# Attention, rational MLP and gated MLP on one core: first q and k loads of one row tile, q's norms summed on columns, and a new order inside the slots of token block 1

## What is computed

```python
qn = q / (norm(q, axis=1) + 1e-06)          # norms over the 6016 rows, one per column
kn = k / (norm(k, axis=1) + 1e-06)
s = kn.transpose(0, 2, 1) @ qn / tau        # 256 x 256
a = softmax(s)                              # the sum has 1e-9 added
x = v @ a                                   # 6016 x 256
h = x @ w_in                                # 6016 x 2048
P = a0 + a1 h + a2 h^2 + a3 h^3
Q = 1 + |b0| |h| + |b1| h^2
y = (P / (Q + 1e-6)) @ w_out                # 6016 x 256
out = (sigmoid(y @ w_gate) * (y @ w_val)) @ w_out2
```

## Time and profile before

| what | value |
|---|---|
| time before, median of 3 runs | 1206.06 us (1205.66 to 1206.26) |
| the profiled execution | 1205.5 us, of which 1203.7 us is its span |
| around the span | 1.8 us |
| PE busy | 1191.9 us, 99% of the span |
| DVE, ACT, POOL busy | 88%, 73%, 21% |
| granted TensorE clock, mean | 1.000 |

### The profile page before, as it was taken

The page is one execution under the profiler, slowest core; times in us unless marked ns, Lnnn a source line. Parts: engine busy times, 40 slices in busy tenths (PEclk is TensorE's granted clock), DMA queues, the critical chain, the costliest instruction groups (busy, mean ns, idle before and its releaser), DMA issues.

```text
span 1203.7 us, 19532 instructions
## 1 busy us (share of the span) xinstructions
PE 1191.9 (99%) x6772; PEld 1165.5 (97%) x6772; DVE 1064.7 (88%) x1369; ACT 881.3 (73%) x1267; POOL 253.8 (21%) x152
## 2 busy tenths in 40 slices
PE   9998999999999999999999999999999999999998
PEld 8876999999999999999999999999999999999998
DVE  7799999899999989999998999899898989989843
ACT  6898778677777868777786877778687777768632
POOL 0432212112121212212121211212121221212110
PEclk9999999999999999999999999999999999999999
DMA  9820000000000000000000000000000000000000
GB/s 368 300 66 13 1 14 14 13 13 0 13 13 13 13 13 13 0 13 13 13 13 13 13 0 13 13 13 13 13 13 0 13 13 13 13 0 13 0 14 14
DMA packets 15866, 33.81 MB, mean 28 GB/s; under 512 B 1382, under 2 KB 6246, under 8 KB 15846
## 3 DMA queue, kind: packets, MB, share of 16 engines
q1 hardware_dynamic: 14982, 32.51, 7.5%
q10 hardware_dynamic: 864, 1.05, 0.3%
HBM read 27.39 MB, written 6.16 MB: 28 GB/s over the span
## 4 chain that ended last, share of the span: by engine, by line
PE 90%; DVE 5%; DMA 2%; SPq 1%; issue 1%; ACT 1%; DVEq 0%; ACTq 0%
PE ps L905 17%; PE ps L903 17%; PE ps L904 17%; PE ps L1017 7%; PE ps L1018 7%; PE ps L1019 7%; PE ps L1056 5%; PE ps L1058 5%; PE ps L1057 5%; DMA kq<-in_q 2%; PE ps L917 1%; SPq L340 1%; SPq L342 1%; PE ps L940 1%; DVE work L875 0%
## 5 line engine op out<-in xcount | busy, mean ns | idle before, releaser
L453 POOL TENSOR_TENSOR g_parts<-work,g_parts 128x752 fp32r<-128x752 f32 x120 | 218.7, 1822 | 814.4 <-ACT g_parts L634 814.4
L624 ACT ACTIVATE work<-ps,neg_a 128x752 f32<-128x752 f32 x120 | 117.6, 980 | 143.5 <-PE ps L905 82.1
L903 PE MATMUL ps<-v_hi,m_hi 128*128 128x376 f32 x512 | 174.1, 340 | 1.2 <-DVE work L862 1.0
L905 PE MATMUL ps<-v_hi,m_lo 128*128 128x376 f32 x512 | 171.5, 335 | 0.0
L904 PE MATMUL ps<-v_lo,m_hi 128*128 128x376 f32 x512 | 170.4, 333 | 0.0
L1017 PE MATMUL ps<-g_parts,w_hi 128*128 128x376 f32 x480 | 160.7, 335 | 0.0
L1018 PE MATMUL ps<-g_parts,w_hi 128*128 128x376 f32 x480 | 160.0, 333 | 0.0
L1019 PE MATMUL ps<-g_parts,w_lo 128*128 128x376 f32 x480 | 159.4, 332 | 0.0
L748 DVE TENSOR_TENSOR work<-work,ps 128x376 f32<-128x376 f32 x192 | 103.7, 540 | 52.6 <-PE ps L905 39.8
L856 DVE TENSOR_TENSOR work<-work,ps 128x752 f32<-128x752 f32 x120 | 112.0, 934 | 37.7 <-ACT work L627 36.0
L660 ACT ACTIVATE work<-work,consts 128x752 f32<-128x752 int32 x118 | 108.4, 918 | 38.7 <-DVE work L875 38.7
(11 more groups left out here) (131 smaller groups left out, 2862.8 us busy)
## 6 DMA issues: line engine op xcount, KB each, us to landing
work<-in_v SPq DMA_DIRECT2D x16, 376.0 KB, 2.9
out<-work SPq DMA_DIRECT2D x15, 376.0 KB, 2.3
kq<-in_k SPq DMA_DIRECT2D x9, 512.0 KB, 13.2
kq<-in_q SPq DMA_DIRECT2D x9, 512.0 KB, 15.5
before<-in_moe_w_out SPq DMA_DIRECT2D x5, 512.0 KB, 12.6
before<-in_moe_w_in SPq DMA_DIRECT2D x8, 256.0 KB, 7.1
before<-in_moe_w_gate SPq DMA_DIRECT2D x2, 512.0 KB, 9.5
before<-in_moe_w_val SPq DMA_DIRECT2D x2, 512.0 KB, 6.7
```

Source lines behind the costliest of these rows:

```text
L453: nc.gpsimd.tensor_tensor(g_lo[n], g[n], as_f32(g_hi[n]), ALU.subtract).then_inc(g_lo_ready, 1)
L624: nc.scalar.activation(poly[n], h, ACT.Identity, scale=neg_a[:, 3:4], bias=neg_a[:, 2:3])
L903: nc.tensor.matmul(dst, l_hi, r_hi, start=(begins and n == 0), stop=False)
L905: last = nc.tensor.matmul(dst, l_lo, r_hi, start=False, stop=(ends and n == len(parts) - 1))
```

## The change

1. `KQ_SIZES` becomes six chunks of one tile, one of two, one of three, nine of four: 17 chunks. ACT still issues the first six q chunks, which are now six tiles and not eight. The coefficients are issued behind the chunk of two tiles, and are spread before the same tile as before.
2. `norms()` moves four late scores back (`NORMS_AT` = 37) and puts q's norms on columns as well: four narrow products instead of two narrow ones and a wide one. ACT takes one root of 128 x 4. DVE adds the guard to q's two columns, takes their reciprocals, and multiplies the identity matrix by each column (two 128 x 128 products). PE spreads the diagonal over all partitions with a product by ones (`spread_q`, before late score 40), and DVE copies the row out of PSUM.
3. In slots 2 to 6 of block 1, `times_value(*second)` moves from the end of DVE's slot to right behind L862, ahead of `split_gated` and `quad`; and `gate(*second)` moves on ACT ahead of L641.
4. In slots 2 to 7 of block 1 ACT computes |h| before the polynomial's start, and so waits for g only after |h|.

```diff
-    KQ_SIZES = [1] * 4 + [2] * 2 + [4] * ((NT - 8) // 4)
-    KQ_SIZES[6:6] = [NT - sum(KQ_SIZES)]
+    KQ_SIZES = [1] * 6 + [2] + [4] * ((NT - 8) // 4)
+    KQ_SIZES[7:7] = [NT - sum(KQ_SIZES)]
...
-    COEF_SPREAD_BEFORE = 9
+    COEF_SPREAD_BEFORE = 10
...
-    NORMS_AT, TURN_AT = NT - 14, NT - 2
+    NORMS_AT, SPREAD_AT, TURN_AT = NT - 10, NT - 7, NT - 2
...
+        def second_ahead(i, j, second):
+            return is_block(i, 1) and second is not None and j < PAIRS - 1
...
             act.wait_ge(norms_summed, 1)
-            nc.scalar.activation(q_inv, ps_qnorm, ACT.Sqrt).then_inc(norms_squared, 1)
-            nc.scalar.activation(k_norm, ps_knorm, ACT.Sqrt).then_inc(norms_squared, 1)
+            nc.scalar.activation(norms_kq, ps_norms, ACT.Sqrt).then_inc(norms_squared, 1)
             act.wait_ge(norms_squared, 1)
-            nc.scalar.activation(q_inv, q_inv, ACT.Identity, bias=norm_guard).then_inc(norms_rooted, 1)
-            act.wait_ge(norms_squared, 2)
...
                     if now is not None:
+                        h = hidden_of(i, j)
                         act.wait_ge(h_done, now + 1)
...
+                        if is_block(i, 1) and j >= 2:
+                            wait_count(act, quad_ready, now)
+                            nc.scalar.activation(ab, h, ACT.Abs)
+                            act.wait_ge(g_ready, now - 1)
+                            nc.scalar.activation(poly[n], h, ACT.Identity, scale=neg_a[:, 3:4],
+                                                 bias=neg_a[:, 2:3]).then_inc(h_read, 1)
...
+                    if second_ahead(i, j, second):
+                        gate(*second)
...
+            dve.wait_ge(norms_squared, 1)
+            link(nc.vector.tensor_scalar(q_inv, q_inv, 1e-6, None, ALU.add))
+            link(nc.vector.reciprocal(q_inv, q_inv))
+            dve.wait_ge(ident_ready, 1)
+            for c in range(CC):
+                nc.vector.tensor_scalar(q_diag[:, c, :], ident[:], q_inv[:, c:c + 1], None,
+                                        ALU.mult).then_inc(q_diag_ready, 1)
             dve.wait_ge(norms_rooted, 1)
-            link(nc.vector.reciprocal(q_inv, q_inv))
-            dve.wait_ge(norms_rooted, 2)
             link(nc.vector.reciprocal(k_inv, k_norm))
...
                 if c == 0:
+                    dve.wait_ge(q_row_ready, 1)
+                    link(nc.vector.tensor_copy(q_row, ps_qrow))
                     dve.wait_ge(first_scores, 1)
...
+                    if second_ahead(i, j, second):
+                        times_value(*second)
                     if j > 0 and left is not None:
                         split_gated(*left)
...
+            def spread_q():
+                pe.wait_ge(q_diag_ready, CC)
+                nc.tensor.matmul(ps_qrow, ones[:], q_diag.rearrange("p a b -> p (a b)"), start=True,
+                                 stop=True).then_inc(q_row_ready, 1)
```

More of the change, by code:

```diff
@@ L163, in attention_rational_gated_kernel @@
         assert 4 * KQ_W <= 6 * PW
-        q_inv = region(6 * PW, (C,))
+        q_row = region(6 * PW, (C,))
+        q_diag = region(6 * PW + 5 * C, (CC, P))
         att = region(6 * PW + C, (CC, C))
@@ L176, in attention_rational_gated_kernel @@
         neg_min, row_sum, row_inv = small[:, 6:8], small[:, 8:10], small[:, 10:12]
+        norms_kq, q_inv = small[:, 12:16], small[:, 14:16]
         consts = sb("consts", [P, 7])
@@ L189, in attention_rational_gated_kernel @@
         ps_kq = ps[:, 0:2, 0:C]
-        ps_knorm, ps_qnorm = ps[:, 2, 0:CC], ps[:, 3, 0:C]
+        ps_norms, ps_qrow = ps[:, 2, 0:2 * CC], ps[:, 5, 0:C]
         ps_coef = ps[:, 4, 0:7]
@@ L204, in attention_rational_gated_kernel @@
         norms_summed, norms_rooted, small_step = sem("norms_summed"), sem("norms_rooted"), sem("small_step")
+        q_diag_ready, q_row_ready = sem("q_diag_ready"), sem("q_row_ready")
         scores_ready, exps_ready, row_inv_ready = sem("scores_ready"), sem("exps_ready"), sem("row_inv_ready")
@@ L506, in _ @@
             act.wait_ge(norms_summed, 1)
-            nc.scalar.activation(q_inv, ps_qnorm, ACT.Sqrt).then_inc(norms_squared, 1)
-            nc.scalar.activation(k_norm, ps_knorm, ACT.Sqrt).then_inc(norms_squared, 1)
+            nc.scalar.activation(norms_kq, ps_norms, ACT.Sqrt).then_inc(norms_squared, 1)
             act.wait_ge(norms_squared, 1)
-            nc.scalar.activation(q_inv, q_inv, ACT.Identity, bias=norm_guard).then_inc(norms_rooted, 1)
-            act.wait_ge(norms_squared, 2)
             act.wait_ge(coefs_ready, 1)
-            nc.scalar.activation(k_norm, k_norm, ACT.Identity, scale=neg_tau,
+            nc.scalar.activation(k_norm, norms_kq[:, 0:CC], ACT.Identity, scale=neg_tau,
                                  bias=neg_tau_guard).then_inc(norms_rooted, 1)
@@ L620, in step @@
                     if now is not None:
+                        h = hidden_of(i, j)
                         act.wait_ge(h_done, now + 1)
[L622 to L627, removed]
+                        if is_block(i, 1) and j >= 2:
[4 more added lines that the diff above has]
+                                                 bias=neg_a[:, 2:3]).then_inc(h_read, 1)
+                        else:
+                            act.wait_ge(g_ready, now - 2 if is_block(i, 1) and j < 2 else now + (-1))
+                            nc.scalar.activation(poly[n], h, ACT.Identity, scale=neg_a[:, 3:4],
+                                                 bias=neg_a[:, 2:3])
+                            wait_count(act, quad_ready, now)
+                            nc.scalar.activation(ab, h, ACT.Abs).then_inc(h_read, 1)
                     if old is not None and not unsplit(old):
@@ L652, in step @@
                     gate_first = is_block(i, 1) and second is not None
-                    if gate_first:
+                    if gate_first and not second_ahead(i, j, second):
                         gate(*second)
@@ L732, in _ @@
                 link(nc.vector.scalar_tensor_tensor(out=att[:, c, :], in0=ps_kq[:, c, :], scalar=k_inv[:, c:c + 1],
-                                                    in1=q_inv, op0=ALU.mult, op1=ALU.mult))
+                                                    in1=q_row, op0=ALU.mult, op1=ALU.mult))
                 nc.vector.tensor_reduce(neg_min[:, c:c + 1], att[:, c, :], AX_X, ALU.min).then_inc(scores_ready, 1)
@@ L887, in step @@
                         split_gated(*early)
-                    if second is not None:
+                    if second is not None and not second_ahead(i, j, second):
                         times_value(*second)
@@ L923, in norms @@
                 pe.wait_ge(summed, 2 * (len(KQ_CHUNKS) + 3))
[L924 to L928, removed]
+                for n in range(2 * CC):
+                    acc, c = (k_acc, q_acc)[n // CC], n % CC
+                    last = nc.tensor.matmul(ps_norms[:, n:n + 1], acc[:, 0, c * P:(c + 1) * P], ones[:, 0:1],
+                                            start=True, stop=True)
+                last.then_inc(norms_summed, 1)
+            def spread_q():
+                pe.wait_ge(q_diag_ready, CC)
+                nc.tensor.matmul(ps_qrow, ones[:], q_diag.rearrange("p a b -> p (a b)"), start=True,
+                                 stop=True).then_inc(q_row_ready, 1)
             def spare_products(count, dst=ps_spare):
@@ L964, in _ @@
                     norms()
+                if late == SPREAD_AT:
+                    spread_q()
                 if late == TURN_AT:
```

## The result

| | median, us | lowest to highest | ratio to before, 95% interval |
|---|---|---|---|
| before (7 runs) | 1205.75 | 1205.42 to 1206.26 | |
| after (7 runs) | 1210.22 | 1209.78 to 1210.90 | 1.0039 (1.0029 to 1.0048) |
| predicted | 1204.6 | 1203.6 to 1208.0 | |

The change makes the kernel 0.4% slower, and the time lies outside the predicted range. The profiled execution took 1210.9 us, 1209.1 of them its span, 5.4 us more than the span of before. It is the longest of the seven, and its mean granted clock, 0.997, is the lowest (0.998 or 0.999 in the other six), so the trace shows a little more loss than the medians, which differ by 4.5 us. I look first at the page, where PE and its chain look nearly as they did.

What follows compares the result with a forecast made beforehand. PE, busy 99% of the span, bounds the kernel, with DVE bounding slots 3 to 6 of block 1. Head 0.3 plus block 1 1.1 saves 1.4 us: 1205.5 to 1204.1, median 0.56 above, so 1204.6; range 1203.6 to 1208.0.

Steps and rivals of the forecast that it cites:

- rival 1 in its second form: Head: POOL holds the guard and diagonal products and gets in between the two; diagonal at 49.8, 1210 us; chance 0.14.
- 1.0 us predicted for the late scores: Head, PE's saving from loads and norms: 1.1 plus 0.4 less 0.5 for added instructions, if the chain isn't later.
- PE's gap of 1.10 us: Head, PE's wait ahead of the norms at 41.27; four more late scores, 1.73 us of work, were to cover it.
- 0.1: Head: the wait the first turn may have, with 2.2 us of scores against a chain of some 2.0 + 0.5.
- the loads' 0.4: Head: smaller first q loads let PE wait less for the eighth tile, 0.4 us, bounds nothing to 1.1.
- the head's 0.3 us: Head: what is left of the late scores' gain once ACT waits for the w_val load; bounds 0.1 to 0.9.
- 0.9: Head: how much sooner all late scores were to be done, in us, before the w_val load takes most back.
- The w_val load: Head: it lands at about 51.05 and ACT's rounding of it delays M's tile 2, leaving 0.3 us, not 0.9.
- the rival in the expectation: Head, written for the run with smaller loads only: the eleventh tile becomes the wait, PE wins nothing; no chance given.
- Block 1: 1.1 us predicted: Block 1: L770 no longer held by POOL, slots of 7.33 us, 0.96; slot 7's sigmoid wait gone, 0.2; bounds 0.2 to 1.5.
- no wait in slot 7: Block 1, slot 7: L748's 0.22 us wait for the sigmoid goes, as \|h\| is done before g arrives; worth 0.2.
- PE's last gap 0.49 us (0.5 written): End of block 1: the new profile would show a PE gap at about 160 us, 0.5 us long.

Runs made afterwards that it cites:

- Experiments 2, 3 and 4: Each on the changed kernel: POOL's subtractions wait for the diagonal, 1204.84 us; diagonal products read the identity from PSUM, 1205.69; one diagonal operation instead of two, 1208.25.
- pool_behind_diagonal: The changed kernel, with POOL starting its four weight subtractions only when the diagonal is written: 1204.84 us.
- block 1's part alone: The kernel before with only the block 1 edits (second value product and its sigmoid ahead, \|h\| ahead): 1204.36 us.
- the third kernel of experiment 6: The changed kernel with guard and diagonal products on ACT, third weight chunk rounded ahead of the roots, spread and first turn one late score later: 1204.26 us.
- the loads' part alone: The kernel before with only the smaller first loads: 1205.24 us.
- the norms' part alone: The kernel before with only q's norms on columns (norms, diagonal, spread, copy, at the new places): 1208.01 us, ratio 1.0031.

## Why the prediction was wrong

**The step that failed** is the cost of the new chain from root to diagonal: a guard at 0.2 us and two products at 0.2 each, priced by a row of before in which a reciprocal of 128 x 2 ran beside POOL in 0.17 us. The reciprocals beside POOL are not held, then or now (0.15 to 0.17 us); a tensor_scalar between SBUF operands is. The guard took 0.78 us and the two products 4.42, so that the diagonal was ready at 48.9 and PE, which wanted it at 44.2, waited 4.73 us where the prediction had no wait. This was rival 1 in its second form, to which I gave 0.14. Its mechanism was right in each part: the guard until POOL's first operation ends, the first product until its second, POOL's third in between the two. Experiments 2, 3 and 4 show it by taking away POOL's work, the SBUF operand and the gap between the products. The Trainium skill, page "SBUF — State Buffer", section "Who interferes with whom", says that the port pair is held for the whole instruction and that the second to ask is blocked; the traces agree with it (0.48 us against 4.42), and with its remark that ACT is not concerned (0.69 us beside POOL). Page "VectorE: DVE Perf Modes" of the Trainium skill, section "Mode 2×_2P — use both read ports for one tensor", wants the operands in SBUF for the form that takes the pair; the run with the identity in PSUM agrees (0.61 us beside POOL). Before had rows on both sides, none of them of this form: L875 and L770, with two SBUF inputs, held, and the reciprocal free. I let the size decide between them, 128 x 2 being nearest to the guard, where the form of the instruction decides; the page named the form.

**Rival 1's time of 1210 came out right by luck, from errors that cancel.** It had the diagonal ready at 49.8; it was ready at 48.9, since POOL's first operation ended at 44.2 and not 44.6 and the products' own time did not come on top of the holds. And it had no term for the clock. It also started from 1206.06, where before's seven runs have a median of 1205.75. From pool_behind_diagonal to after, the spread moves by 48.96 - 44.24 = 4.72 us, and from the spread to the third M tile it takes 8.96 us instead of 6.79: 2.2 us more, which is the halved clock less the 0.43 us wait before the turn that the slow scores now cover. 4.72 + 2.17 - 0.25 = 6.64. That is the profiled execution; by the mean clocks of the other six, their second bill was probably smaller.

**Norms without the stall: 1.0 us predicted for the late scores, 0.25 measured.** Of the terms, PE's gap of 1.10 us went, and PE waited only 0.18 us for the diagonal. But the first turn waits 0.43 us and not 0.1 (the exponential comes 2.9 us behind the spread, with 2.4 us of scores to cover it), and the loads' 0.4 didn't come to pass here: PE came to the norms at 41.89, where 40.17 + 1.73 = 41.90 was its old place. So the head's 0.3 us was met with 0.25 by luck: the prediction reached it as 0.9 less what the w_val load takes back, and here there was no 0.9 to take from. Nor does a median show the 0.25: the kernels without the stall, 1204.26 to 1204.84, lie around block 1's part alone, 1204.36. What the norms on columns are worth was not shown by any run.

**The w_val load** did not set the head's end, in any run. After the change, with the diagonal on ACT, it was issued at 40.54 and landed 10.0 us later, at 50.5, not at the 51.05 of the prediction; ACT rounded its half from 51.08, straight behind its own work. In the third kernel of experiment 6 it was issued at 41.06 and so landed at about 51.1, but the split behind ACT's rounding still waited 0.16 us for PE. The rule that it caps the head's gain at 0.3 us was not tested, since no kernel had more to give there.

**Smaller loads: 0.4 predicted, not seen in the time** (1205.24 against 1205.55, an interval that holds 1). The prediction looked at the sixth and eighth tile only. Of the nine traces with the new loads eight have a wait for q of 0.36 to 0.39 us between 11.4 and 12.0 us, and none of the five with the old ones does: part of the wait has moved to a later tile, which was the rival in the expectation. What the traces show is how much this place varies: taking PE's own wait or the four scores out, it is ready for the norms at 40.1 to 41.2 us in the five traced kernels with the loads of before, and at 39.9 to 40.6 in the nine with the new ones. The means are 40.6 and 40.2, which so few single executions can't tell apart; in before and in the loads' part alone the norms come at 41.27 and 41.28, because there DVE's last sum (L719) releases them.

**Block 1: 1.1 us predicted, 1.25 in the trace after, 1.2 as a part alone.** Slots of 7.32 us, the gated tile's rest at 0.54, no wait in slot 7, PE's last gap 0.49 us (0.5 written): each as forecast. What I didn't see is that the two edits are not two gains: |h| ahead carries it, the value product alone brings nothing.

## What to carry to other kernels

Before a short operation is put on DVE beside a running POOL, look not at its size but at its form: two of 128 x 128 cost 4.4 us here, and on ACT 0.7 or from PSUM 0.6. Two such operations in a row were two holds here, since POOL's next operation got in between. And a stall of PE can have a second bill, paid behind it at half clock: here 2.0 us on a stall of 4.7, 1.3 on one of 3.3, 1.4 on one of 5.1, and none on one of 1.75. It differs between executions of one kernel, so a single trace can over- or understate it.

## What was unexpected of the hardware

- A guard add on 128 x 2 elements is held like a wide operation: 0.78 to 1.61 us, 0.17 without POOL.
- A wait of PE of 3.3 us (one diagonal operation) brought the granted clock to 0.50 for about 3.4 us, one of 4.7 us for almost 7 us, one of 5.1 us (the norms' part alone) again for only 3.4 us, one of 1.75 us not at all, and 36 spare weight loads in the wait kept it at 1.00.
